# Routing of a mixture-of-experts block: once for 512 tokens instead of once for each 128

## The reference

```
h = x @ w_in                                   # 512 -> 2048
g = (a0 + a1 h + a2 h^2 + a3 h^3) / (1 + |b0||h| + |b1| h^2 + 1e-6)
x2 = g @ w_out                                 # 2048 -> 512
```

```
logits = x2 @ w_gate                           # 512 -> 8
expert_idx = argmax(logits, axis=1)
gate_w = softmax(logits) at expert_idx
out[token] = gate_w * (relu(x2 @ w1[e]) @ w2[e])   # e = expert_idx of the token
```

## Time and profile before

| | |
|---|---|
| median of 3 timed runs | 1014.97 us (1014.4 to 1017.12) |
| the profiled execution's own time | 1013.33 us |
| its span, first to last instruction | 1011.7 us |
| TensorE busy | 988.0 us (98%) |
| weight loads / VectorE / ScalarE / POOL busy | 809.5 / 649.7 / 580.4 / 403.3 us |

### The profile page before, as it was taken

One profiled execution on the slowest core, in us unless ns is written; L12 is line 12 of the kernel. 1 busy time (PEld: TensorE's weight loads), 2 busy tenths in 40 slices (PEclk: granted clock), 3 DMA queues, 4 the chain that ended last, 5 costly groups with the idle time before them and its releaser, 6 DMA issues.

```text
span 1011.7 us, 19801 instructions
## 1 busy us (share of the span) xinstructions
PE 988.0 (98%) x6190; PEld 809.5 (80%) x6191; DVE 649.7 (64%) x1242; ACT 580.4 (57%) x1277; POOL 403.3 (40%) x388
## 2 busy tenths in 40 slices
PE   7888999999999999999999999999999999999997
PEld 5776778888888888888888888887888888888886
DVE  6878788778876886787678778864523523425222
ACT  6878787776676676667667677742523324325221
POOL 3677354544544455455445545623111211112111
PEclk9999999999999999999999999999999999999999
DMA  8999702950692097029101021104721511511100
GB/s 318 331 395 368 291 32 89 361 187 12 213 365 80 10 324 248 0 89 357 53 10 42 16 89 63 63 11 164 251 95 36 207 42 53 186 42 45 39 31 26
DMA packets 58033, 142.48 MB, mean 141 GB/s; under 512 B 4663, under 2 KB 10423, under 8 KB 57984
## 3 DMA queue, kind: packets, MB, share of 16 engines
q1 hardware_dynamic: 51120, 121.03, 34.3%
q0 software_dynamic: 6560, 20.77, 6.0%
q10 hardware_dynamic: 304, 0.04, 0.0%
HBM read 70.29 MB, written 72.32 MB: 141 GB/s over the span
## 4 chain that ended last, share of the span: by engine, by line
PE 88%; DVE 4%; ACT 4%; issue 2%; DMA 1%; POOL 1%; POOLq 0%; ACTq 0%; DVEq 0%
PE PS L679 25%; PE PS L517 25%; PE PS L551 15%; PE PS L560 13%; ACT prob L877 2%; PE PS L544 2%; PE PS L699 2%; DVE PS L1074 1%; PE PS L623 1%; PE PS L534 1%; PE PS L507 1%; PE PS L719 1%; DVE rsafe L1083 1%; PE PS L593 1%; DVE prob_t L1067 1%
## 5 line engine op out<-in xcount | busy, mean ns | idle before, releaser
L517 PE MATMUL PS<-xs,weights 128*128 (+1 forms) x1152 | 282.7, 394 | 0.0
L517 PEld LDWEIGHTS PS<-xs,weights 128*128 128x128 f32 x1152 | 212.6, 188 | 43.1
L679 PE MATMUL PS<-weights,g_hi 128*128 128x512 f32 x768 | 238.0, 391 | 1.2 <-POOL g_lo L1445 0.7
L1445 POOL TENSOR_TENSOR g_lo<-g_sb,g_hi 128x512 fp32r<-128x512 f32 x96 | 124.4, 1296 | 275.1 <-ACT g_hi L965 272.7
L679 PEld LDWEIGHTS PS<-weights,g_hi 128*128 128x128 f32 x768 | 143.0, 188 | 35.0 <-issue 2.9
L679 PE MATMUL PS<-weights,g_lo 128*128 128x512 f32 x384 | 149.6, 390 | 0.0
L946 ACT ACTIVATE b_ln<-PS,cf 128x512 f32<-128x512 f32 x96 | 66.0, 688 | 141.3 <-PE PS L517 141.3
L560 PE MATMUL PS<-weights,h_hi 128*128 (+1 forms) x432 | 136.0, 396 | 1.3 <-DVE h_lo L1141 1.2
L551 PE MATMUL PS<-weights,xg_hi 128*128 (+1 forms) x432 | 136.0, 396 | 0.5 <-issue 0.5
L1448 POOL TENSOR_TENSOR den<-den,b_r 128x512 f32<-128x512 f32 x96 | 128.9, 1343 | 2.1 <-ACT b_r L973 2.1
L1187 DVE SCALAR_TENSOR_TENSOR den<-den,b_r 128x512 f32<-128x512 f32 x96 | 65.9, 686 | 49.0 <-POOL den L1448 48.8
(11 more groups left out here) (196 smaller groups left out, 1584.7 us busy)
## 6 DMA issues: line engine op xcount, KB each, us to landing
rows_by_expert<-pad_rows SPq DMA_DIRECT2D x16, 1799.0 KB, 20.8
e_raw<-w_exp SPq DMA_DIRECT2D x34, 512.0 KB, 5.7
qk<-qk_all SPq DMA_DIRECT2D x32, 480.0 KB, 7.0
rows_by_expert<-pad_rows SPq DMA_DIRECT2D x8, 1542.0 KB, 20.2
vw<-v_all SPq DMA_DIRECT2D x32, 384.0 KB, 6.8
rows_by_expert<-pad_rows SPq DMA_DIRECT2D x8, 1285.0 KB, 18.7
w_raw<-w_mlp SPq DMA_DIRECT2D x16, 512.0 KB, 8.0
pad_rows<-rows_by_expert POOLq DMA_DIRECT2D x27, 257.0 KB
```

The costliest lines, as they stand in the source:

```text
L517: last = pe.matmul(PS[:, H_BANK + f % 2, :], w[:, wp], rhs, start=k == 0, stop=k == 3 * KT - 1)
L679: last = pe.matmul(PS[:, ACC_BANK + s, :], gp[:, f % 2, s * P:(s + 1) * P], w[:, wp], start=f == 0 and k == 0, stop=f == FT - 1 and k == 2)
L1445: pool.tensor_tensor(g_lo[:, q], g_sb[:], g_hi[:, q].bitcast(F32), ALU.subtract).then_inc(g_lo_done, 1)
```

## The change

Routing of block i-1 is done once for its 512 tokens in steps 3 to 15 of block i, for blocks 1 to 5:

- The gate's weights are split once, in the attention part, into upper and lower parts side by side: `wg_split`, 16 columns for each of four depth slices.
- In steps 3 to 6 TensorE transposes one depth slice of x2 for all 512 tokens (four transposes into bank 6). In the step after each, ScalarE writes the upper part `x2t_hi`, VectorE the lower `x2t_lo`, and TensorE, at the end of that step, streams both over the 16 gate columns, accumulating in partitions 0 to 15 of bank 7.
- In step 8 ScalarE copies these 16 rows of 512 logits, and TensorE turns them back with four transposes. In step 9 VectorE adds upper and lower, and forms maximum, shift and one-hot rows for 4 x 8 values a partition at once; gate values follow in step 10, ranks in step 10 (14 bf16 matmuls), positions in step 11, the four indirect writes in steps 12 to 15.
- In block 5 the second fetch moves from step 9 to 11, and the first tile's transposes from step 4 to 9.
- Padding between tiles in SBUF goes or changes, and some tiles change places.

```
-LAG_XT, LAG_XT_COPY, LAG_LOGITS, LAG_HOT, LAG_RANK, LAG_POS, LAG_ROWS = 3, 4, 4, 5, 6, 7, 8
+XT_STEP, LOGIT_STEP, TURN_STEP, HOT_STEP, GATE_STEP, RANK_STEP, POS_STEP, ROWS_STEP = 3, 4, 8, 9, 10, 10, 11, 12
+def routes_at(st, step):
+    return st.m == step and not st.in_period(0) and not st.in_period(BLOCKS)
+def route_part(st, first):
+    k = st.m - first
+    return k if 0 <= k < SUBS and not st.in_period(0) and not st.in_period(BLOCKS) else None
...
+            with ExitStack() as over:
+                turn = sb("turn", [P, TB], F32, over)
+            x2t_hi = sb("x2t_hi", [P, TB], F32R, ph)
+            x2t_lo = sb("x2t_lo", [P, TB], F32R, ph)
... TensorE
-                if r := route_step(st, LAG_RANK):
-                    pe.wait_ge(hot_ready, r[1] + 1)
...
-                    pe.matmul(PS[:, 6, 2 * E:3 * E], tri[:], hot[:, r[0] % 2, :], start=True, stop=False, skip_group_check=True)
-                    pe.matmul(PS[:, 6, 2 * E:3 * E], ones[:], seen[:], start=False, stop=True,
-                              skip_group_check=True).then_inc(rank_ready, 1)
-                if r := route_step(st, LAG_LOGITS):
-                    pe.wait_ge(x2t_copied, r[1] + 1)
-                    for kt in range(KT):
-                        last = pe.matmul(PS[:, 6, 0:E], x2_t[:, kt, :], wg_sb[:, kt, :], start=kt == 0, stop=kt == KT - 1,
-                                         skip_group_check=True)
-                    last.then_inc(logits_ready, 1)
+                if routes_at(st, RANK_STEP):
+                    pe.wait_ge(hot_ready, st.i)
+                    pe.wait_ge(seen_done, upto(seen_done, st.i - 1))
+                    for s in range(SUBS):
+                        at = PS[:, 6, RANKS + s * E:RANKS + (s + 1) * E]
+                        pe.matmul(at, tri[:], hot[:, s], start=True, stop=False, skip_group_check=True)
+                        for k in range(s):
+                            pe.matmul(at, ones[:], hot[:, k], start=False, stop=False, skip_group_check=True)
+                        last = pe.matmul(at, ones[:], seen[:], start=False, stop=True, skip_group_check=True)
+                    last.then_inc(rank_ready, 1)
+                if (kt := route_part(st, LOGIT_STEP)) is not None:
+                    done = st.i * KT - KT + kt
+                    if kt == 0:
+                        pe.wait_ge(turn_copied, upto(turn_copied, st.i - 1))
+                    pe.wait_ge(x2t_copied, done + 1)
+                    pe.matmul(PS[0:2 * E, 7, :], wg_split[:, kt, :], x2t_hi[:], start=kt == 0, stop=False, skip_group_check=True)
+                    pe.wait_ge(x2t_lower, upto(x2t_lower, done + 1))
+                    pe.matmul(PS[0:2 * E, 7, :], wg_split[:, kt, :], x2t_lo[:], start=False, stop=kt == KT - 1,
+                              skip_group_check=True).then_inc(logits_ready, 1)
+                if routes_at(st, TURN_STEP):
+                    pe.wait_ge(turn_copied, upto(turn_copied, st.i))
+                    for s in range(SUBS):
+                        last = pe.transpose(PS[:, 6, s * P:(s + 1) * P], turn[:, s * P:(s + 1) * P], ident)
+                    last.then_inc(turn_ready, 1)
...
+                    pe.wait_ge(x2t_lower, upto(x2t_lower, done))
+                    for s in range(SUBS):
+                        last = pe.transpose(PS[:, 6, s * P:(s + 1) * P], x2[:, s, kt * P:(kt + 1) * P], ident)
... ScalarE
+                if (kt := route_part(st, LOGIT_STEP)) is not None:      # before b_ln
+                    act.activation(x2t_hi[:], PS[:, 6, :], ACT.Copy).then_inc(x2t_copied, 1)
+                if routes_at(st, TURN_STEP):
+                    act.activation(turn[0:2 * E, :], PS[0:2 * E, 7, :], ACT.Copy).then_inc(turn_copied, 1)
... VectorE, between g_sb and den
+                if (kt := route_part(st, LOGIT_STEP)) is not None:
+                    dve.wait_ge(x2t_copied, done + 1)
+                    dve.wait_ge(logits_ready, upto(logits_ready, done))
+                    dve.tensor_tensor(x2t_lo[:], PS[:, 6, :], x2t_hi[:].bitcast(F32), ALU.subtract).then_inc(x2t_lower, 1)
+                if routes_at(st, HOT_STEP):
+                    chain(dve.tensor_copy(lg[:], turned[:, :, E:2 * E]))
+                    chain(dve.tensor_tensor(lg[:], lg[:], turned[:, :, 0:E], ALU.add))
+                    chain(dve.tensor_reduce(one[:, 0], lg[:], AX.X, ALU.max))
+                    dve.tensor_tensor(sh[:], lg[:], each_of(0), ALU.subtract).then_inc(logits_read, 1)
+                if routes_at(st, GATE_STEP):
+                    ...                                                 # five small operations
... POOL
+                if (k := route_part(st, ROWS_STEP)) is not None:
+                    if k == 0:
+                        pool.wait_ge(cleared, ...)
+                        pool.wait_ge(row_ready, st.i)
+                    send_rows(k)
...
-F_AT = (2, 9)
-X_AT = (4, 4, 5)
+F_AT = (2, 11)
+X_AT = (9, 9, 10)
```

More of the change, by code:

```diff
@@ L226, in build @@
         iota = cst[:, C_IOTA:C_IOTA + P]
-        sb("before_x", [P, PAD_RAW])
+        place = sb("place", [P, SUBS], U32)
+        hot = sb("hot", [P, SUBS, E], BF16)
+        sh, ex, pick = (sb(n, [P, SUBS, E]) for n in ("sh", "ex", "pick"))
         pad_rows = sb("pad_rows", [P, ROW_SB])
@@ L261, in build @@
             x2 = sb("x2", [P, SUBS, XW], F32, ph)
[L262 to L271, removed]
+            lg = sb("lg", [P, SUBS, E], F32, ph)
+            posx = sb("posx", [P, 2, SUBS, E], F32, ph)
+            one = sb("one", [P, 6, SUBS], F32, ph)
+            with ExitStack() as over:
+                turn = sb("turn", [P, TB], F32, over)
+            x2t_hi = sb("x2t_hi", [P, TB], F32R, ph)
+            x2t_lo = sb("x2t_lo", [P, TB], F32R, ph)
             early = sb("early", [P, 2, E], F32, ph)
+            count = sb("count", [P, E], F32, ph)
         with ExitStack() as ph:
@@ L705, in _ @@
                     pe.matmul(PS[:, 6, 0:E], ones[:], seen[:], start=True, stop=True, skip_group_check=True).then_inc(early_counts, 1)
-                if st.in_period(BLOCKS - 1) and st.m == LAG_XT:
+                if st.in_period(BLOCKS - 1) and st.m == XT_STEP:
                     pe.wait_ge(first_ready, 1)
                 if st.in_period(BLOCKS - 1) and st.m == X_AT[0]:
+                    pe.wait_ge(turn_copied, upto(turn_copied, BLOCKS - 1))
                     transpose_x(0)
[L710 to L719, removed]
+                if (kt := route_part(st, XT_STEP)) is not None:
+                    done = st.i * KT - KT + kt
+                    if kt == 0:
+                        pe.wait_ge(acc_act, st.i * 2)
+                        pe.wait_ge(acc_dve, st.i * 2)
+                        pe.wait_ge(rank_read, upto(rank_read, st.i - 1))
+                    pe.wait_ge(x2t_lower, upto(x2t_lower, done))
+                    for s in range(SUBS):
+                        last = pe.transpose(PS[:, 6, s * P:(s + 1) * P], x2[:, s, kt * P:(kt + 1) * P], ident)
@@ L1040, in setup @@
                 chain(dve.memset(seen[:], 0.0))
-                chain(dve.tensor_scalar(tok[:], cst[:, C_TOK:C_TOK + 1], -float(P), None, ALU.add))
+                chain(dve.tensor_scalar(tok[:], cst[:, C_TOK:C_TOK + 1], -float(TB), None, ALU.add))
             def refine_root():
@@ L1091, in _ @@
                     refine_root()
+                if d == 5:
+                    dve.wait_ge(wg_upper, 1)
+                    dve.tensor_tensor(wg_split[:, :, E:], wg_sb[:], wg_split[:, :, 0:E].bitcast(F32),
+                                      ALU.subtract).then_inc(wg_lower, 1)
             then = Chain(dve, first_chain)
@@ L1155, in _ @@
             chain = Chain(dve, route_chain)
+            four_of = lambda x: x.unsqueeze(1).to_broadcast([P, SUBS, E])
+            each_of = lambda k: one[:, k].unsqueeze(2).to_broadcast([P, SUBS, E])
             for st in pipelined(dve, BLOCKS, FT, 1):
@@ new lines, in _ @@
+                if routes_at(st, POS_STEP):
+                    dve.wait_ge(rank_read, upto(rank_read, st.i))
+                    dve.wait_ge(hot_ready, st.i)
+                    chain(dve.tensor_reduce(count[:], hot[:].rearrange("p s e -> p e s"), AX.X, ALU.add))
+                    dve.tensor_tensor(seen[:], seen[:], count[:], ALU.add).then_inc(seen_done, 1)
+                    chain(dve.tensor_tensor(posx[:, 1], posx[:, 0], hot[:], ALU.mult))
+                    chain(dve.tensor_reduce(one[:, 2], posx[:, 1], AX.X, ALU.add))
+                    dve.tensor_copy(place[:], one[:, 2]).then_inc(row_ready, 1)
```

105 lines of the change are left out of this document (43 added, 62 removed).

## The result

In six runs of each kernel on one chip the median went from 1014.68 to 1008.48 us, ratio 0.9935 [0.9915, 0.9956], 6.2 us less. Five more runs later, beside nine of the kernel before, gave 1007.67 against 1015.3, ratio 0.9922 [0.9909, 0.9936], 7.6 us less. The forecast was 1007.0. By its interval the change makes the kernel faster.

What follows compares the result with a forecast made beforehand. TensorE, busy 98% of the span, was taken as the bound; -8.3 us in blocks 1 to 5 and +0.3 setup gave -8.0, so 1007.0 us as a median, range 1004.8 to 1012.

Steps and rivals of the forecast that it cites:

- TensorE sets the time: Blocks 1 to 5: TensorE's chain has no hole, so routing falls from 6.25 to 4.59 us a block, saving 8.3.
- The narrow weights load beside the stream: Logits in blocks 1 to 5: 8 matmuls at 0.227 us, 1.81 a block; bounds 0.227 to 0.578 each.
- rival 1: Narrow logits matmuls drain TensorE at both edges, 0.163 us each, 6.5 in all: 1013.5 us; chance 0.10.
- Where the gain is: TensorE's routing: old logits about 3.9 us a block; new logits 1.81, transposes back 0.46, ranks 0.48, x2 transposes unchanged.
- VectorE's x2t_lo costs nothing: VectorE between g_sb and den: 0.69 us subtractions, wanted by TensorE about 1.3 us later, costed at nothing.
- The idle time of 0.64: VectorE's wait for ScalarE before den, expected to absorb x2t_lo's 0.69 us, leaving den some 0.1 us later.
- Sends: Indirect writes moved to steps 12 to 15: last packets down 1.7 us before block 2's accumulator copies, no wait.
- Rival 3: Sends queue under clears, landing 3 us later, TensorE late in step 2, VectorE's chain late: 1011.0 us; chance 0.12.
- Setup: Attention part: two small operations, on ScalarE and VectorE, add 0.3 us together.
- The total: Whole kernel: -8.3 + 0.3 = -8.0 us, to a median of 1007.0 us; forecast's chance 0.71.

Runs made afterwards that it cites:

- the doubled pair: Changed kernel with each pair of logits matmuls issued twice, 16 instead of 8 narrow matmuls a block; block 93.56 or 93.53 us, 1.82 more.
- the narrow turn: Changed kernel with the four transposes back made of 16 rows only, behind one added small matmul; 1008.16 us, ratio to kernel before 0.9923.
- Batching alone: Changed kernel's schedule with old operands (float32 tokens loaded, 8 gate columns streamed); 1013.48 us, ratio to kernel before 0.9982.

## Why the prediction was right

- **TensorE sets the time.** Right. In blocks 1 to 5 it was, before and after, without a hole, and what was taken from its instructions came off the time: 1.6 us a block of 1.66 forecast, 7.9 of 8.3 in all. Step lengths forecast as 5.90, 6.35, 5.89, 5.90, 5.44, 5.90 and 5.44 (steps 3, 4 to 6, 7, 8, 9, 10, 11) are 5.80, 6.36 to 6.37, 6.02, 5.81, 5.55, 5.80 and 5.53. The misses of a tenth go both ways and nearly cancel. They have one cause in the main: the 0.10 to 0.12 that a group of transposes, or of ranks, costs in the first product behind it falls into the next step, and I had counted it in the group's own.
- **The narrow weights load beside the stream.** Right, 0.227 us each, the low end of the bounds. The bounds were far apart (0.227 and 0.578), and what chose between them was the nearest row, the second product of the same type with its larger load. The loads of 0.09 us, one matmul ahead, and the doubled pair confirmed it. My argument against rival 1 was weaker than I thought: that records overlap doesn't show that nothing is lost. At the place that I read the earlier trace rows, the starts say that something is:

```profile
63.84 0.25 PE L593 MATMUL PS<-qk 64*64 64x96 f32 x4
64.02 0.31 PE L610 MATMUL PS<-cst,prob 128*96 128x128 f32 x1
```

  The groups of four in 64x64 tiles follow each other every 0.08 us, and then 0.18 pass before the first transpose, at least 0.17 in all 28 such places of the trace; the narrow turn lost about as much at its edges. That weights of 16 columns have no such edge was measured only afterwards: there the forecast had luck.
- **Where the gain is.** Right in its sum, wrong in its parts. By the forecast the operands gave 3.9 - (1.81 + 0.46) = 1.6 us a block and batching next to nothing (ranks 0.53 before, 0.48 after). Batching alone gave 0.45, and the operands 1.2 on top. The 0.97 that I booked as the products' own holds also what a group of its own costs the product behind it (3.03 instead of 2.88), and that part goes as soon as logits and transposes stand together.
- **VectorE's x2t_lo costs nothing.** Right in its result, and wrong in its reason. The 1.3 us (1.9 measured) is the slack of one instance; a delay in each of four steps isn't made up between them, and the slack is then that of the ring, 6.36 - 5.46 = 0.9 us. The idle time of 0.64 in which I had placed the 0.69 is now 0.47, behind it. One more operation of 0.7 us beside it costs nothing, two more cost 3.1 a block.
- **Sends.** Right that they cost nothing, wrong in the margin: forecast 1.7 us, measured none (0.17 us of waiting). I had shifted one send's landing by a step and kept the time from issue to landing, and this time grew. In the kernel before the packets lay between 288.0 and 290.1, up to 5.3 us behind the issue's end (284.75); now they lie between 292.5 and 296.1, up to 7.0 us behind it (289.09). Of the 80, 77 are down by 295, and three stragglers hold the landing up for another microsecond. The sends are one step apart now instead of two; that this is what stretches them was not tested. From 292 to 297 us:

```profile
q1 hardware_dynamic: 665, 1.34, 89.3%
q0 software_dynamic: 80, 0.26, 15.2%
```

  The clears fill 89% of the DMA engines' time there. Rival 3 named this place; it put 3 us on the landing, and the margin shrank by 1.9. In one block of the kernel with batching alone, which sends in the same steps, it did cost TensorE 0.42 us.
- **Setup.** +0.3 forecast. The part ahead of the 80 steps was 187.32 and 187.79 before and 187.63 to 188.23 in the changed kernel (three profiles): right in size, hardly more than the scatter.
- **The total.** -8.0 forecast; -7.6 in the larger comparison, -6.2 in the first. In the profiles of that first one the difference of 2 us is the experts' part, which differs by 2.7 and 2.5 us between two profiles of the same kernel. That the 1.4 us between the two comparisons is this as well was not shown; their intervals overlap.

## What to carry to other kernels

A product whose stationary operand is a tile of tokens and whose moving operand has 8 columns costs its load, 0.23 us each here; with the operands exchanged, the split into two and the transposes back can still be cheaper, and the measured distance between the starts of like matmuls tells so in advance. Read costs at an edge between shapes from these starts too, not from records that overlap. The slack of an operation that recurs in each step is not its distance from who waits for it, but the step less the length of the ring through it; look for that ring before adding to it. When transfers are moved closer together, their landing times don't shift with them one for one.

## What the runs showed of the hardware, not expected

- Transposes of 16x128 pieces follow each other at 0.07 us instead of 0.11, but lose about 0.1 us at each edge to 128-row work, so that four of them gain nothing. Weights of 16 columns over all 128 rows lose nothing at their edges.
- POOL's cast of 128x1, 0.19 us alone, takes 0.21 to 2.42 us beside VectorE's splits with two inputs in SBUF: it ends 0.04 to 0.05 us behind the end of a split, sometimes the second or third. The longest made TensorE wait 1.22 us.
- The other way round, a VectorE operation of 0.69 us with two inputs in SBUF that starts while POOL's 128x512 subtraction has more than 0.4 us to run ends 0.55 us behind it, up to 1.74 us long. One with an input in PSUM isn't held.
- An indirect write of 80 packets, issued by 289.1 us, was moved between 292.5 and 296.1: over 3 us before it begins and nearly 4 for 0.26 MB, among clears that hold 89% of the DMA engines.
